# Second coarse scores one slot sooner, and a window's values loaded ahead of the next raw keys, in a fused attention and two-layer kernel

## The reference

```python
# 1: attention, coarse (groups of 4 positions averaged, 144 of them) plus local (|i - j| < 4)
out_d = sm_attn(mean4(q), mean4(k), mean4(v));  out_up = repeat(out_d, 4)
scores = where(|i - j| < 4, q @ k.T / 8, -1e9)
x = transpose(out_up + softmax(scores) @ v)          # (4, 576, 512)
# 2: layer norm, 512 -> 2048 -> 512 with relu, residual
x = x + relu(layernorm(x) * g @ w_ch1) @ w_ch2
# 3: mix with the previous position, then gate
k_ = relu((mu_k*x + (1-mu_k)*x_prev) @ w_k);  v_ = (k_*k_) @ w_v
out = sigmoid((mu_r*x + (1-mu_r)*x_prev) @ w_r) * v_
```

## Time and profile before

| | |
|---|---|
| median of 3 runs | 782.68 us (781.73 to 785.26) |
| the profiled execution's own time | 782.57 us |
| its span in the profile | 780.7 us |
| PE busy | 755.7 us (97%) |
| PEld busy | 693.8 us (89%) |
| DVE busy | 433.0 us (55%) |
| ACT busy | 269.5 us (35%) |
| POOL busy | 225.2 us (29%) |

### The profile page before, as it was taken

How to read it: one execution, slowest core, us unless ns; L and a number is a source line. 1 busy time by engine, 2 the same in 40 slices (tenths; PEclk the granted TensorE clock), 3 DMA queues, 4 the chain that set the end, 5 groups by cost and what they waited for, 6 DMA issues and landing times.

```text
span 780.7 us, 15717 instructions
## 1 busy us (share of the span) xinstructions
PE 755.7 (97%) x6412; PEld 693.8 (89%) x6412; DVE 433.0 (55%) x797; ACT 269.5 (35%) x640; POOL 225.2 (29%) x260
## 2 busy tenths in 40 slices
PE   5799999999999999999999999999999999999997
PEld 5589999999999999989999999998888888888886
DVE  5967654434654344553443433466687576766655
ACT  5655422223123223223222321455433434423322
POOL 5266654133343224434312313003111111111101
PEclk9999999999999999999999999999999999999999
DMA  9982441220441022252011001731103002010010
GB/s 193 235 271 45 95 90 29 51 64 7 81 94 39 13 55 55 46 96 57 10 29 39 2 14 34 274 109 35 51 1 108 1 9 72 1 55 1 0 55 28
DMA packets 117959, 49.67 MB, mean 64 GB/s; under 512 B 96640, under 2 KB 106880, under 8 KB 117888
## 3 DMA queue, kind: packets, MB, share of 16 engines
q1 hardware_dynamic: 117888, 48.68, 24.9%
HBM read 39.20 MB, written 9.45 MB: 62 GB/s over the span
## 4 chain that ended last, share of the span: by engine, by line
PE 90%; SPq 3%; ACT 2%; issue 2%; DVE 2%; DMA 1%; POOL 0%; POOLq 0%; DVEq 0%; ACTq 0%
PE psH L955 26%; PE psY L972 23%; PE psH L1006 12%; PE psY L1025 12%; PE psA L988 6%; SPq L533 2%; PE psA L872 2%; PE psA L903 2%; PE psA L820 1%; ACT prob L1099 1%; PE psA L848 1%; PE psA L833 1%; PE psA L883 1%; DMA v_win<-in_v_dram 1%; DMA k_first<-in_k_dram 0%
## 5 line engine op out<-in xcount | busy, mean ns | idle before, releaser
L1565 DVE SCALAR_TENSOR_TENSOR h_lo<-psH,h_hi 128x288 fp32r<-128x288 f32 x128 | 58.4, 456 | 202.3 <-ACT h_hi L1273 202.3
L972 PE MATMUL psY<-h_hi,w_hi 128*128 128x288 f32 x512 | 158.5, 310 | 0.1
L955 PE MATMUL psH<-xc_hi,w_hi 128*128 128x288 f32 x512 | 156.1, 305 | 2.4 <-DVE xc_lo L1437 2.4
L955 PE MATMUL psH<-xc_lo,w_hi 128*128 128x288 f32 x512 | 152.2, 297 | 0.0
L955 PE MATMUL psH<-xc_hi,w_lo 128*128 128x288 f32 x512 | 151.8, 297 | 0.0
L972 PE MATMUL psY<-h_hi,w_lo 128*128 128x288 f32 x512 | 150.9, 295 | 0.0
L972 PE MATMUL psY<-h_lo,w_hi 128*128 128x288 f32 x512 | 150.9, 295 | 0.0
L1273 ACT ACTIVATE h_hi<-psH 128x288 fp32r<-128x288 f32 x128 | 52.5, 410 | 258.2 <-PE psH L955 258.1
L794 POOL TENSOR_TENSOR relu_k<-relu_k 128x512 f32<-128x512 f32 (+1 forms) x40 | 39.0, 975 | 246.9 <-ACT relu_k L1236 246.9
L955 PEld LDWEIGHTS psH<-xc_hi,w_hi 128*128 128x128 f32 x512 | 97.1, 190 | 5.5 <-issue 4.6
L972 PEld LDWEIGHTS psY<-h_hi,w_hi 128*128 128x128 f32 x512 | 96.1, 188 | 3.7 <-issue 1.3
(11 more groups left out here) (169 smaller groups left out, 1333.4 us busy)
## 6 DMA issues: line engine op xcount, KB each, us to landing
w_raw<-in_moe_w_ch_dram SPq DMA_DIRECT2D x8, 1024.0 KB, 7.4
v_win<-in_v_dram SPq DMA_DIRECT2D x84, 56.0 KB
x_scratch<-x SPq DMA_DIRECT2D x8, 576.0 KB, 4.0
out_dram<-gate SPq DMA_DIRECT2D x18, 256.0 KB, 2.2
raw<-in_q_dram SPq DMA_DIRECT2D x112, 36.0 KB, 2.1
raw<-in_k_dram SPq DMA_DIRECT2D x96, 36.0 KB, 1.9
v_raw<-in_v_dram SPq DMA_DIRECT2D x12, 288.0 KB
x_sh<-x_scratch SPq DMA_DIRECT2D x3, 1026.0 KB, 5.5
```

The source lines that it names most:

```text
L955: ins = mm(psH[:, m % 2, 0:N], ws[a][:, kt, f * P:(f + 1) * P], xx[bb][:, kt], start=(kt == 0 and i == 0), stop=(kt == KT - 1 and i == 2))
L972: ins = mm(psY[:, d, 0:N], ws[a][:, f, d * P:(d + 1) * P], hs[bb][:, m % 2], start=(f == 0 and i == 0), stop=(f == NF1 - 1 and i == 2))
L1565: nc.vector.scalar_tensor_tensor(out=h_lo[:, m % 2], in0=psH[:, m % 2, 0:N], scalar=0.0, in1=h_hi[:, m % 2].bitcast(F32), op0=ALU.max, op1 ...
```

## The change

The second coarse scores (`Sd` 1) move from slot 5 to slot 4 of each unit (for unit 1 from slot 7 to slot 6), so on TensorE from behind `down_b` to ahead of it; the parts on VectorE, ScalarE and GpSimd that hang on its slot by their lags move one slot too. `PdT` stays in slot 7. On SP, within a slot, `load_window` is issued ahead of `load_later`.

```diff
     SLOTS = 2 * NF1
     LEAD = 24
-    LATER = [(2, "Sd", 0), (5, "Sd", 1),
+    LATER = [(2, "Sd", 0), (4, "Sd", 1),
              (7, "PdT", 0), (8, "S", 0), (10, "PdT", 1), (12, "S", 2), (13, "OD", 0),
...
             for slot in range(-LEAD, SLOTS * NU):
                 if slot in V_LOAD:
                     load_v_sum(*V_LOAD[slot])
-                for x_ in flips_at(slot):
-                    if HALF <= flip_of[x_] < len(flips) - RAW:
-                        load_later(flip_of[x_] + RAW)
                 for kind, u, n in steps_at(slot):
                     for part in parts_of(kind, u, n):
                         if kind == "AV" and NW_U * u + part + 2 < NWIN:
                             load_window(NW_U * u + part + 2)
+                for x_ in flips_at(slot):
+                    if HALF <= flip_of[x_] < len(flips) - RAW:
+                        load_later(flip_of[x_] + RAW)
```

## The result

| | kernel before | changed kernel |
|---|---|---|
| median | 783.8 us (781.73 to 785.26, 4 runs) | 777.04 us (776.63 to 777.88, 4 runs) |
| ratio | | 0.9917, 95% interval 0.9889 to 0.9945 |
| the profiled execution, its span | 782.57 us, 780.7 us | 776.8 us, 774.9 us |

The change is 0.8% faster. 776.5 was forecast, and a gain of 6.1 us; the ratio makes it 6.5 (4.3 to 8.7), the two profiled executions 5.8.

What follows compares the result with a forecast made beforehand. PE was taken as the bound, busy 755.7 of 780.7 us, so only its waits count. Scores 5.32 - 2.01 = 3.31 us plus window 2.77 make 6.08 off 782.57: 776.5 us, range 774.6 to 779.3.

Steps and rivals of the forecast that it cites:

- The transposes' wait: PE at L833, `PdT` 0 waiting for `exp_d` 1 in units 1 to 7: goes whole, 5.32 us.
- The worry that `norm_d` 0 takes its place: At L833, the wait goes over to `norm_d` 0, so only the window's part comes: 779.8 us, chance 0.03.
- The new wait at slot 4: PE at L820, `Sd` 1 waiting for `exp_d` 0: loses 0.71 us in unit 2, 0.26 in units 3 to 7, 2.01 together.
- the third rival: Slower: at `Sd` 1 in slot 4, any slip of `exp_d` 0 stands on PE's path; 784.3 us, chance 0.03.
- The window's values: PE at L903, waits for the DMA into v_win in windows 1 and 2: both go whole, 2.77 us.
- The cover: Window loads of slots 80 and 144: with SP's order turned, data are ready 2.9 and 3.5 us before PE comes.
- the second rival: At L903, transfers ahead of the window, not SP's issue, keep it late: 779.3 us if all is lost, chance 0.05.
- the sum: Whole kernel: 3.31 us from the scores plus 2.77 from the window, 6.08 off 782.57, so 776.5 us.

Runs made afterwards that it cites:

- slot 3 kernel: The changed kernel with `Sd` 1 one slot sooner still, at slot 3 in place of slot 4; 793.73 us, ratio 1.0126 to the kernel before.

## Why the prediction was right

**The transposes' wait** (5.32 us to be had): right. `PdT` 0 of unit 5 starts 5.53 us after `Sd` 1 and in unit 1 also 5.53, with no wait at L833 in any of the seven units. The worry that `norm_d` 0 takes its place was unfounded; in unit 5 it runs from 297.28 for 1.15 us, and `PdT` 0 starts at 300.74.

**The new wait at slot 4** (2.01 us): right in place and cause, and to 0.01 us in units 3 to 7. In unit 2 it was 0.71 in the prediction and 0.44 here (109.86 - 105.40 - 4.02), 0.57 in the second profile of the changed kernel, 0.49 with the scores moved alone. The flip that delays DVE there waited for its raw queries 0.91, 1.05 and 0.96 us in these three and not the 1.20 of the earlier trace rows, so this term hangs on DMA and is no constant. All six waits came to 1.74 us and not 2.01. The slot 3 kernel shows what the third rival's place is worth when it does decide: the whole wait, and in three of six cases 1.5 us on top, at a granted clock of 0.50.

**The window's values** (2.77 us): right, 2.8 alone by the ratio and 2.7 by the profile. The cover was ample: the four DMAs end their issue at 201.15, PE could begin some 1.74 later as in the prediction, and it reads at 206.20. What the second rival feared, transfers ahead that hold the window, cost nothing here: with the coarse values sent right ahead of it, the window of the changed kernel was in time, and in the kernel before its last load landed 1.94 to 2.35 us after its issue began, about as a raw load does. No row shows the window held by transfers sent ahead of it; a hold that ends within this time is neither shown nor ruled out.

**What the sum left out.** From unit 1's first scores to the end of the span the two profiles differ by 6.2 us, the whole spans by 5.8. The missing 0.4 lies ahead of unit 1: `Sd` 0 is at 47.03 where it was at 46.64. There TensorE is still slow: the granted clock is 0.50 from 20 to 43 us, and the matmuls of 128x288 stand 0.24 us apart until 43.1 us, and until 42.0 in the profile of before. The edits touch nothing up to there, and the place varies by execution: 46.01 to 46.92 in the three further profiles of the kernel before, 47.36 in the second of the changed kernel, 46.16 to 48.31 with one edit alone. So the forecast of 776.5 against the profiled 776.8 is closer than its terms: unit 2's wait stood in the sum 0.27 too high, and the 0.4 ahead of unit 1 was not in it. That they partly cancel is luck.

The other way, the kernel before has executions some 2 us longer that the changed kernel hardly has (785 against at most 777.9). That is why its median beside the change is 783.8 and the gain 6.5, more than the 6.1 worked out from an execution without that. The removal of waits of 1.5 us and more as the cause is only argued.

## What to carry to other kernels

Measure a wait from start to start against the same step where it doesn't wait; the idle time in brackets was 0.07 to 0.17 us short of the loss here, and over the seven waits of the transposes that makes 4.2 us of 5.3. When a step is moved ahead to relieve its successor, look at once at what it now waits for itself: here a slot won 0.60 us a unit behind it and lost 0.26 ahead of it, and the next slot sooner lost 1.6 and more. With many small DMAs the engine that issues them can be what is short: here each took SP 0.45 to 0.65 us (1.80 us for four, 5.21 for eight). So order them by who is waited for first.

## What the runs showed of the hardware

- A wait of 1.8 to 1.9 us in a stream of matmuls was followed in three of six cases by some 3 us at a granted clock of 0.50, worth 1.5 us; behind waits of 0.2 to 0.5 us no such fall was seen, nor behind those of 0.9 to 2.0 us in four profiles of the kernel before, by the clock (1.00) or by the durations of the matmuls. The same wait cost 1.8 us or 3.3.
- The granted clock's row can hide this: in the kernel before it reads 1.00 from 37 to 42 us, where the matmuls of 128x288 take 0.44 us and start 0.24 apart, as in the changed kernel at a granted 0.50. So the mean granted clock of an execution isn't sure to hold its start.

```profile
37.00:42.00 5.00, 4.38 (x18) 4.42 (x19) 4.39 (x9) 3.15 (x7) 3.52 (x3) 1.00 1.03 321
```
```profile
37.00:43.00 6.00, 5.51 (x23) 5.54 (x24) 5.39 (x10) 4.03 (x8) 3.55 (x4) 0.50 0.92 254
```

The first is the kernel before, the second the changed kernel, both as stretches: 18 matmuls in 5 us against 23 in 6, about the same pace, where the slot 3 kernel's stretch at a granted 1.00 above has 35 in 4.
